# Moving the first products with v, the division and the MLP groups in an attention and mixture-of-experts kernel

## The chip, the cores and the metric

The kernel runs on one core of a Trainium2 chip. The metric is the device time of one execution in microseconds (us). A core has five engines that run their own instruction streams and meet through semaphores: TensorE (PE in the profile, its weight loads PEld) multiplies matrices, VectorE (DVE) and ScalarE (ACT) work on tiles and empty the accumulators (PSUM), GpSimd (POOL) works on tiles in SBUF, SyncE (SP) issues transfers (DMAs). Each engine works through its stream in the order in which the program writes it: an instruction that waits holds up all that stand behind it on that engine.

## The reference, cut to what matters

```python
# attention: B, H, S, D = 4, 8, 576, 64; a query sees the keys of its own and earlier blocks of 64
scores = q @ k.T / sqrt(D)          # masked with -1e9
attn   = exp(scores - max); attn /= attn.sum(-1) + 1e-9
x      = (attn @ v)                 # then laid out as 2304 tokens x 512
# first MLP, 512 -> 2048 -> 512
h = x @ w_in; x2 = maximum(0.01 * h, h) @ w_out
# mixture of experts, 8 experts, 512 -> 1024 -> 512, one expert a token, or none
out = x2;  out[t] += gate[t] * (relu(x2[t] @ w1[e]) @ w2[e])
```

## The kernel before

The change lies in the first of three stages, which takes the first 298 us: attention, with a part of the first MLP between its pieces so that TensorE has work while other engines answer. Then follow the rest of the MLP and the experts, which the change leaves as they are.

Attention runs over 16 pairs of heads. A pair has nine units of query rows: for either head the query tiles 0 to 3 (128 to 512 score columns), and between them, as unit 4, the tail of both heads (576 columns). For each unit PE makes the scores (`scores`, line 1598), DVE takes the maximum (line 1249), ACT the exponentials with their sums (`exponential`, line 1025), PE turns the result (`transposes`, line 1631), DVE or for units 3 and 8 ACT copies the turned tile out (`copy_turned`, lines 1252 and 1074). Per pair, PE multiplies with v in two halves (`p_v`, line 1643), both in one PSUM bank `ps_o`; DVE copies each half out (`copy_o`, line 1269); the sums' reciprocals are turned on PE (`turn_inverse`, line 1671, into that bank too, so it waits for the first half's copy), copied, stored by SP and spread over the partitions by SP (`spread_inverse`, line 670). POOL divides (`normalise`, line 865), ACT takes the high part (`high_x`, line 1013) and POOL the low part (`low_x`, line 872) of the quotient for the MLP. From pair 6 on, keys too are split in a high and a low part: DVE makes the high part, POOL the low part of the lower half (`low_k`, line 857), and SP copies the high part beside it (`copy_k`, line 662, DMA at 664); the scores of units 0 and 4 wait for both.

The MLP's first product is cut into groups of 12 matmuls, in two parts of 6 (`hidden`, line 1677), each product taken three times with high and low parts. Groups 0 to 31 have 512 columns, 32 to 47 have 256. A group is accumulated in a PSUM bank, ACT copies it out (`copy_hidden`, line 1042), SP stores it (`store_hidden`, line 694). Until group `TWO_BANKS` all groups share one bank, so a group's first matmul waits until ACT has copied the one before (`hidden_waits`, line 1689). Group 0 waits for pair 3's low part, and group 48, the first behind attention, for the last pair's.

The order is written out by hand as 156 steps, one for each unit and twelve more. `fill_steps` (line 118) says in which step each group's parts stand. Up to step 85 (`DOUBLE` is 86) PE does in step s the scores of unit s+2, the transposes of unit s-2, the products with v if it is their turn, and the group's part if there is one. From step 86 on two steps are taken at a time (a double step, named here by its first, as D118): PE does the scores of s+2 and s+3, the transposes of s-2 and s-1, the products with v, then the group. ACT, DVE, POOL and SP walk over the same steps; SP's loop stores in step s the groups that step s-1 completed, behind that step's other transfers.

Of the kernel before, what the change touches and what calls it, by code (L numbers as in the profile page):

```python
# [75 lines left out]
TWO_BANKS = 2 * FC + 8  # L76
# [41 lines left out]
def fill_steps():  # L118

    at = {s: [] for s in range(STEPS)}  # L120
    for g in range(N_ATT_HID):
        for part in range(2):
            if g < FC:
                s = 50 + 34 * (2 * g + part) // (2 * FC)
            elif g < 2 * FC:
                s = DOUBLE + 34 * (g - FC) // FC
            elif g < TWO_BANKS:
                s = 122 + 22 * (g - 2 * FC) // (TWO_BANKS - 2 * FC)
            else:
                s = N_UNITS + 5 + 7 * (g - TWO_BANKS) // (N_ATT_HID - TWO_BANKS)  # L130
            at[s].append((g, part))
    return at
# [13 lines left out]
def head_step(s):  # L146


    return divmod(s, UNITS) if s < DOUBLE else divmod(s - 1, UNITS) if s > DOUBLE else (N_PAIRS, 0)

# [83 lines left out]
def build(nc, q_t, k_t, v_r, w_in, w_out, w_gs, w1, w2, out):  # L234
    ctx = ExitStack()
    with ctx:
# [575 lines left out]
        def _(e):  # L812
# [74 lines left out]
            for s in range(STEPS):  # L887
# [7 lines left out]
                if i == 7 and 1 <= p <= N_PAIRS:  # L895
                    normalise(p - 1)
                if i == (3 if p < ROW_PAIRS else 1) and 2 <= p <= N_PAIRS + 1:
                    low_x(p - 2)
# [104 lines left out]
        def _(e):  # L1003
# [77 lines left out]
            def between(s):  # L1081
# [7 lines left out]
                if i == (2 if p < ROW_PAIRS else 0) and 2 <= p <= N_PAIRS + 1:  # L1089
                    high_x(p - 2)  # L1090
# [4 lines left out]
            for s in range(DOUBLE + 2):  # L1095
                if s >= 3 and s - 3 < DOUBLE - 2 and (s - 3) % UNITS in by_act((s - 3) // UNITS):
                    copy_turned(s - 3)
                if s <= DOUBLE:
                    for g in filled_at(s - 1):
                        copy_hidden(g)  # L1100
                exponential(s)
                between(s)
# [113 lines left out]
        def _(e):  # L1216
# [106 lines left out]
            for s in range(DOUBLE, STEPS, 2):  # L1323
                for u in (s + 2, s + 3):
                    if u < N_UNITS:
                        maximum(u)
                for u in (s - 2, s - 1):
                    if u < N_UNITS and u % UNITS not in by_act(u // UNITS):
                        copy_turned(u)
                for u in (s, s + 1):  # L1330
                    p, i = divmod(u, UNITS)
                    part = p_v_at(u)
                    if part and part[3] == (QT if part[1] else 2):
                        copy_o(part[0], part[1])
# [229 lines left out]
        def _(e):  # L1564
# [160 lines left out]
            for s in range(DOUBLE, STEPS, 2):  # L1725
# [4 lines left out]
                for g in before:  # L1730
                    for part in range(2):
                        hidden(g, part)
                for u in (s - 2, s - 1):
                    if u < N_UNITS:
                        transposes(u)
                products_with_v(s)
                products_with_v(s + 1)
# [258 lines left out]
```

How the kernel before makes its waits and increments, by code:

```python
        def turned(e, u):  # L541
            p, i = divmod(u, UNITS)
            act_done = 2 * p + sum(k <= i for k in by_act(p))
            dve_done = (UNITS + 1) * p + i + 1 + (i > TAIL) - act_done
            if act_done:
                e.wait_ge(s_pta, act_done)
            if dve_done:
                e.wait_ge(s_ptd, dve_done)
# [20 lines left out]
        def turned_ready(e, u):  # L570
            p = u // UNITS
            e.wait_ge(s_ptr, u + 1)
            if p >= 2:
                e.wait_ge(s_pv, 2 * (p - 1))
# [4 lines left out]
        def loaded_to(e, x, n):  # L580
            for k, loaded in enumerate(s_w[x % NW]):
                e.wait_ge(loaded, 16 * (W_LOADS // 2 * (x // NW) + (n + 2 - k) // 2))
# [1 line left out]
        def loaded_second(e, second, n):  # L585
            for k, loaded in enumerate(s_w[(E - 1) % NW]):
                e.wait_ge(loaded, second * (16 * ((n + 2 - k) // 2)) + 16 * (W_LOADS // 2))
# [19 lines left out]
        def tile_starts(e):  # L608
            e.wait_ge(s_count, 1)
            return [tile_start(e, x) for x in range(E + 1)]
# [7 lines left out]
        def load_q(e, p):  # L618
            if p >= 2:
                e.wait_ge(s_score, UNITS * (p - 1))
            e.dma_start(q_sb[p % 2][:, :], pair_in(q_t, p)).then_inc(s_qk[p % 2], 16)
# [1 line left out]
        def load_k(e, p):  # L623
            if p >= 2:
                e.wait_ge(s_score, UNITS * (p - 1))
            e.dma_start(k_sb[p % 2][:, :], pair_in(k_t, p)).then_inc(s_qk[p % 2], 16)
# [53 lines left out]
            def load_w_in(f):  # L680
                if f == 0:
                    e.wait_ge(s_maskd, 32)
                if f >= 2:
```

## Time and profile before

| | |
|---|---|
| median of 3 runs (lowest, highest) | 763.32 us (762.51, 764.35) |
| the profiled execution's own time | 763.2 us |
| its span | 761.4 us |
| granted TensorE clock | 0.999 of full speed |

The span is the time from the first to the last instruction of the program in the profile. PE's records of matmuls overlap: one with 512 columns is given some 0.39 us, while the next starts 0.23 us later. A stall is therefore better read from one start to the next than from the idle time alone, which counts from the modelled end.

### The profile page before, as it was taken

What the parts mean: (1) busy time and instruction counts of PE and PEld (TensorE: products, weight loads), DVE (VectorE), ACT (ScalarE), POOL (GpSimd) and SP (SyncE); (2) the same over time, 40 slices, a digit from 0 to 9 for tenths busy, and PEclk for the clock granted to TensorE, in tenths of its full rate; (3) what the DMA queues carried; (4) which work ended last, traced back from release to release, by engine and by line L of the source; (5) the groups of instructions that cost most, each with busy time, mean ns of one, the idle gap of its engine ahead of it and who ended that gap; (6) DMA issues with size and microseconds to landing.
All of it is one profiled execution on the core that took longest, in us unless ns stands there. A gap on an engine that the chain in (4) does not pass through costs nothing.

```text
span 761.4 us, 12875 instructions
## 1 busy us (share of the span) xinstructions
PE 741.8 (97%) x4446; PEld 597.1 (78%) x4447; DVE 359.2 (47%) x761; ACT 295.2 (39%) x685; POOL 146.5 (19%) x190
## 2 busy tenths in 40 slices
PE   7999999999999989999999999999999999999997
PEld 4555778778788778888888888888887879999984
DVE  6776454464446650122245455564556252262641
ACT  5566564465355542333322222222222131242550
POOL 3226555233212422000020000000000031212221
PEclk9999999999999999999999999999999999999999
DMA  4335677545554514556556565566653117877771
GB/s 130 115 111 158 201 217 206 155 136 141 148 150 134 158 52 122 171 147 171 159 176 189 153 179 167 186 173 172 173 160 105 56 29 238 255 237 238 229 229 58
DMA packets 97538, 121.62 MB, mean 160 GB/s; under 512 B 13842, under 2 KB 60706, under 8 KB 97480
## 3 DMA queue, kind: packets, MB, share of 16 engines
q1 hardware_dynamic: 94664, 116.50, 52.5%
q0 software_dynamic: 1920, 3.77, 1.6%
q8 instruction: 34, 0.56, 0.3%
q10 hardware_dynamic: 896, 0.59, 0.2%
q14 instruction: 24, 0.20, 0.1%
HBM read 89.09 MB, written 31.31 MB: 158 GB/s over the span
## 4 chain that ended last, share of the span: by engine, by line
PE 93%; issue 2%; ACT 1%; DVE 1%; DMA 1%; POOL 1%; SPq 0%; POOLq 0%; DVEq 0%; ACTq 0%
PE ps_h L1683 9%; PE ps_x L1760 9%; PE ps_h L1685 9%; PE ps_h L1684 9%; PE ps_x L1762 9%; PE ps_x L1761 9%; PE ps_hid L1927 8%; PE ps_o L1666 6%; PE ps_t L1640 4%; PE ps_y L1939 2%; PE ps_y L1940 2%; PE ps_y L1938 2%; PE ps_s L1627 2%; PE ps_s L1628 2%; PE ps_s L1591 1%
## 5 line engine op out<-in xcount | busy, mean ns | idle before, releaser
L1683 PE MATMUL ps_h<-xh,win_h 128*128 128x512 f32 (+1 forms) x320 | 123.4, 386 | 3.1 <-ACT act L1046 2.1
L1685 PE MATMUL ps_h<-xh,win_l 128*128 128x512 f32 (+1 forms) x320 | 118.2, 369 | 0.0
L1684 PE MATMUL ps_h<-xl,win_h 128*128 128x512 f32 (+1 forms) x320 | 118.1, 369 | 0.0
L1760 PE MATMUL ps_x<-wout_h,g_hi 128*128 128x512 f32 x288 | 114.7, 398 | 0.0
L1762 PE MATMUL ps_x<-wout_h,g_lo 128*128 128x512 f32 x288 | 112.4, 390 | 0.0
L1761 PE MATMUL ps_x<-wout_l,g_hi 128*128 128x512 f32 x288 | 112.2, 390 | 0.0
L1032 ACT ACTIVATE prob<-ps_s,neg_max 128x128 f32<-128x128 f32 (+3 forms) x144 | 78.9, 549 | 47.3 <-DVE neg_max L1249 36.2
L1046 ACT ACTIVATE act<-ps_h 128x512 f32<-128x512 f32 (+1 forms) x80 | 44.4, 554 | 135.1 <-PE ps_h L1685 135.0
L1249 DVE TENSOR_REDUCE neg_max<-ps_s 128x1 f32<-128x128 f32 (+3 forms) x144 | 71.1, 510 | 51.5 <-PE ps_s L1628 27.6
L1289 DVE TENSOR_TENSOR g_lo<-g_raw,g_hi 128x512 fp32r<-128x512 f32 x72 | 49.6, 689 | 75.8 <-ACT g_hi L1056 75.7
L1683 PEld LDWEIGHTS ps_h<-xh,win_h 128*128 128x128 f32 x320 | 60.3, 188 | 16.1 <-issue 5.9
L1685 PEld LDWEIGHTS ps_h<-xh,win_l 128*128 128x128 f32 x320 | 60.3, 188 | 10.6
L1684 PEld LDWEIGHTS ps_h<-xl,win_h 128*128 128x128 f32 x320 | 60.4, 189 | 8.5
L1760 PEld LDWEIGHTS ps_x<-wout_h,g_hi 128*128 128x128 f32 x288 | 54.1, 188 | 12.3 <-issue 2.0
L1762 PEld LDWEIGHTS ps_x<-wout_h,g_lo 128*128 128x128 f32 x288 | 54.1, 188 | 11.5
L1761 PEld LDWEIGHTS ps_x<-wout_l,g_hi 128*128 128x128 f32 x288 | 54.1, 188 | 10.4
L1056 ACT ACTIVATE g_hi<-g_raw 128x512 fp32r<-128x512 f32 x72 | 43.6, 629 | 47.4 <-PE ps_x L1762 26.9
L1255 DVE COPY pt<-ps_t 128x384 f32<-128x384 f32 (+4 forms) x113 | 46.7, 433 | 28.3 <-PE ps_t L1640 28.1
L1640 PE MATMUL ps_t<-ident,prob 128*128 128x128 f32 x339 | 54.5, 277 | 0.7 <-DVE pt L1255 0.4
L1284 DVE SCALAR_TENSOR_TENSOR g_raw<-g_raw 128x512 f32<-128x512 f32 x72 | 49.2, 684 | 7.4 <-DMA g_raw<-hidden 7.4
L1666 PE MATMUL ps_o<-pt,v_sb 128*64 128x320 f32 (+4 forms) x448 | 51.7, 365 | 0.0
L1640 PEld LDWEIGHTS ps_t<-ident,prob 128*128 128x128 f32 x339 | 39.7, 141 | 10.9 <-issue 4.1
(205 smaller groups left out, 1077.0 us busy)
## 6 DMA issues: line engine op xcount, KB each, us to landing
g_raw<-hidden SPq DMA_DIRECT2D x72, 256.0 KB, 3.8
hidden<-act SPq DMA_DIRECT2D x64, 256.0 KB, 2.4
w_sb<-in_w SPq DMA_DIRECT2D x32, 512.0 KB, 5.0
w_two<-in_w SPq DMA_DIRECT2D x32, 512.0 KB, 5.2
k_raw<-in_k_t SPq DMA_DIRECT2D x40, 144.0 KB, 3.1
x2rows<-x SPq DMA_DIRECT2D x18, 256.0 KB, 2.4
out<-x SPq DMA_DIRECT2D x18, 256.0 KB, 2.6
w_stage<-in_w_in SPq DMA_DIRECT2D x16, 256.0 KB, 3.2
```

Of the source, the lines that this page charges most:

```text
L1032: e.activation(prob_of(u), score_out(u), ACT.Exp, bias=neg_max[:, u % 4:u % 4 + 1], scale=1.0, accum_out=row_sum[p % 2][:, sum_column(u):s ...
L1249: e.tensor_reduce(out=neg_max[:, u % 4:u % 4 + 1], in_=src, axis=AX.XY if u % UNITS == TAIL else AX.X, op=ALU.max, negate=True).then_inc(s ...
L1289: e.tensor_tensor(g_lo[j % G_RING][:, :, :], g_raw[j % RAW_RING][:, :, :], g_hi[j % G_RING][:, :, :].bitcast(F32), ALU.subtract).then_inc( ...
L1640: last = e.transpose(t_bank(u, P, P * kt, P * kt + P), tile[:, P * kt:P * kt + P], ident[:, :])
L1666: last = e.matmul(ps_o[own, a:a + cols], v_sb[p % 2][:, kt, own], pt[p % 2][:, h, at:at + cols], start=kt == 0, stop=kt == tiles - 1)
L1683: e.matmul(dst, win_h[:, f, kc, :], xh[m][:, kc, :], start=kc == 0, stop=False)
L1684: e.matmul(dst, win_h[:, f, kc, :], xl[m][:, kc, :], start=False, stop=False)
L1685: last = e.matmul(dst, win_l[:, f, kc, :], xh[m][:, kc, :], start=False, stop=kc == KC - 1)
L1760: e.matmul(dst, hi, wout_h[:, f, :], start=f == 0, stop=False)
L1761: e.matmul(dst, hi, wout_l[:, f, :], start=False, stop=False)
L1762: last = e.matmul(dst, lo, wout_h[:, f, :], start=False, stop=f == FC - 1)
L1927: last = e.matmul(ps_hid[half][:, P * f - HALF * half:P * (f + 1) - HALF * half], w1_sb[i][:, c, P * f:P * f + P], rows_t[:, c, :], start= ...
```

## The change

It has five edits. (1) In double steps PE does a pair's first half of the products with v (`first_half`) in front of the transposes, and DVE copies that half out in front of the turned tiles. (2) The first 16 groups begin at step 51 instead of 50 and end at step 84 instead of 82; their parts skip steps 62 and 74 where they skipped 66. (3) `TWO_BANKS` goes from 40 to 44: groups 34 to 43 stand in one double step each (D126 to D144), where D128, D136, D142 and D144 had none, and 44 to 47 are left for the last steps instead of 40 to 47; 40 to 43 use the one bank. (4) Up to step 87 ACT takes a step's exponential in front of the copy of the group that was completed the step before. (5) In double steps POOL's division comes one step later and so behind `low_k`, and high and low part of the quotient one step later too.

```diff
--- before.py
+++ after.py
@@ -73,7 +73,7 @@
 WIDE = (0, 512, 1024, 1280, 1792, 2304)
 N_HID = (len(WIDE) - 1) * FC
 N_ATT_HID = 3 * FC
-TWO_BANKS = 2 * FC + 8
+TWO_BANKS = 2 * FC + 12
 ACT_RING = 3
 PIECE = 4
 PIECES = NT * FC // PIECE
@@ -121,11 +121,11 @@
     for g in range(N_ATT_HID):
         for part in range(2):
             if g < FC:
-                s = 50 + 34 * (2 * g + part) // (2 * FC)
+                s = 51 + 35 * (2 * g + part) // (2 * FC)
             elif g < 2 * FC:
                 s = DOUBLE + 34 * (g - FC) // FC
             elif g < TWO_BANKS:
-                s = 122 + 22 * (g - 2 * FC) // (TWO_BANKS - 2 * FC)
+                s = 122 + 2 * (g - 2 * FC)
             else:
                 s = N_UNITS + 5 + 7 * (g - TWO_BANKS) // (N_ATT_HID - TWO_BANKS)
             at[s].append((g, part))
@@ -147,6 +147,11 @@
 
 
     return divmod(s, UNITS) if s < DOUBLE else divmod(s - 1, UNITS) if s > DOUBLE else (N_PAIRS, 0)
+
+
+def first_half(s):
+
+    return p_v_at(s) is not None and p_v_at(s)[1] == 0
 
 
 def t_index(u):
@@ -892,9 +897,9 @@
                         low_k(2 * hp + 2)
                     if hi == 7:
                         low_k(2 * hp + 3)
-                if i == 7 and 1 <= p <= N_PAIRS:
+                if i == (7 if s < DOUBLE else 8) and 1 <= p <= N_PAIRS:
                     normalise(p - 1)
-                if i == (3 if p < ROW_PAIRS else 1) and 2 <= p <= N_PAIRS + 1:
+                if i == (3 if p < ROW_PAIRS else 1 if s < DOUBLE else 2) and 2 <= p <= N_PAIRS + 1:
                     low_x(p - 2)
                 f, odd = divmod(s - 42, 2)
                 if odd == 0 and 0 <= f < FC:
@@ -1086,7 +1091,7 @@
                         high_q(2 * hp + 2)
                     if hi == 7:
                         high_q(2 * hp + 3)
-                if i == (2 if p < ROW_PAIRS else 0) and 2 <= p <= N_PAIRS + 1:
+                if i == (2 if p < ROW_PAIRS else 0 if s < DOUBLE else 1) and 2 <= p <= N_PAIRS + 1:
                     high_x(p - 2)
                 f, odd = divmod(s - 42, 2)
                 if odd == 0 and 0 <= f < FC:
@@ -1095,10 +1100,10 @@
             for s in range(DOUBLE + 2):
                 if s >= 3 and s - 3 < DOUBLE - 2 and (s - 3) % UNITS in by_act((s - 3) // UNITS):
                     copy_turned(s - 3)
+                exponential(s)
                 if s <= DOUBLE:
                     for g in filled_at(s - 1):
                         copy_hidden(g)
-                exponential(s)
                 between(s)
 
 
@@ -1324,14 +1329,17 @@
                 for u in (s + 2, s + 3):
                     if u < N_UNITS:
                         maximum(u)
+                for u in (s, s + 1):
+                    if first_half(u):
+                        copy_o(p_v_at(u)[0], 0)
                 for u in (s - 2, s - 1):
                     if u < N_UNITS and u % UNITS not in by_act(u // UNITS):
                         copy_turned(u)
                 for u in (s, s + 1):
                     p, i = divmod(u, UNITS)
                     part = p_v_at(u)
-                    if part and part[3] == (QT if part[1] else 2):
-                        copy_o(part[0], part[1])
+                    if part and part[1] and part[3] == QT:
+                        copy_o(part[0], 1)
                     if i == 1 and 1 <= p <= N_PAIRS:
                         copy_inverse(p - 1)
                 between(s + 2)
@@ -1730,11 +1738,16 @@
                 for g in before:
                     for part in range(2):
                         hidden(g, part)
+
+                for u in (s, s + 1):
+                    if first_half(u):
+                        products_with_v(u)
                 for u in (s - 2, s - 1):
                     if u < N_UNITS:
                         transposes(u)
-                products_with_v(s)
-                products_with_v(s + 1)
+                for u in (s, s + 1):
+                    if not first_half(u):
+                        products_with_v(u)
                 for g in behind:
                     for part in range(2):
                         hidden(g, part)
```

Below, what the streams hold at three places. PE at steps 50 to 52: `ps_h` is a group's bank, `ps_t` holds transposes, `ps_s<-k_sb` and `ps_s<-k_st` scores. Before:

```order
L1666 MATMUL ps_o<-pt,v_sb 64x192 x2
L1666 MATMUL ps_o<-pt,v_sb 64x64 x2
L1683 MATMUL ps_h<-xh,win_h 128x512
L1684 MATMUL ps_h<-xl,win_h 128x512
L1685 MATMUL ps_h<-xh,win_l 128x512
L1683 MATMUL ps_h<-xh,win_h 128x512
L1684 MATMUL ps_h<-xl,win_h 128x512
L1685 MATMUL ps_h<-xh,win_l 128x512
L1640 MATMUL ps_t<-ident,prob 128x128 x4
L1591 MATMUL ps_s<-k_sb,q_sb 128x512 x2
L1594 MATMUL ps_s<-mask_k,mask_q 128x64 x2
```

Now:

```order
L1674 MATMUL ps_o<-pt,v_sb 64x192 x2
L1674 MATMUL ps_o<-pt,v_sb 64x64 x2
L1648 MATMUL ps_t<-ident,prob 128x128 x4
L1599 MATMUL ps_s<-k_sb,q_sb 128x512 x2
L1602 MATMUL ps_s<-mask_k,mask_q 128x64 x2
L1691 MATMUL ps_h<-xh,win_h 128x512
L1692 MATMUL ps_h<-xl,win_h 128x512
L1693 MATMUL ps_h<-xh,win_l 128x512
L1691 MATMUL ps_h<-xh,win_h 128x512
L1692 MATMUL ps_h<-xl,win_h 128x512
L1693 MATMUL ps_h<-xh,win_l 128x512
L1635 MATMUL ps_s<-k_st,q_hi 128x128
```

The first part of group 0 has moved behind step 51's scores, and the first scores with split keys (`k_st`) now follow one part and not two.

SP at steps 130 to 136: `k<-k_st` is `copy_k`, `hidden<-act` a group's store, `v_sb` the last load of v. Before:

```order
L664 DMA k<-k_st 64x576
L676 DMA inv_all<-inverse 64x576
L677 DMA inv_all<-inverse 64x64
L678 DMA inv_all<-inverse 64x512
L698 DMA hidden<-act 128x2x128
L655 DMA v_sb<-in_v_r 128x4x128
L657 DMA v_sb<-in_v_r 64x128
L664 DMA k<-k_st 64x576
L698 DMA hidden<-act 128x2x128 x2
```

Now:

```order
L669 DMA k<-k_st 64x576
L681 DMA inv_all<-inverse 64x576
L682 DMA inv_all<-inverse 64x64
L683 DMA inv_all<-inverse 64x512
L703 DMA hidden<-act 128x2x128
L660 DMA v_sb<-in_v_r 128x4x128
L662 DMA v_sb<-in_v_r 64x128
L703 DMA hidden<-act 128x2x128
L669 DMA k<-k_st 64x576
L703 DMA hidden<-act 128x2x128 x2
```

The store of group 37 now stands in front of the last `copy_k`.

ACT from D140 to the end of attention: `xh<-inv_all` is `high_x`, `act<-ps_h` the copy of a group, `pt<-ps_t` the copy of a turned tile. Before:

```order
L1046 ACTIVATE act<-ps_h 128x256
L1032 ACTIVATE prob,row_sum<-ps_s,neg_max 128x512
L1023 ACTIVATE row_sum<-row_sum 128x9
L1018 ACTIVATE xh<-inv_all 128x64
L1018 ACTIVATE xh<-inv_all 128x512
L1077 ACTIVATE pt<-ps_t 128x4x128
L1046 ACTIVATE act<-ps_h 128x256 x3
```

Now:

```order
L1051 ACTIVATE act<-ps_h 128x256
L1037 ACTIVATE prob,row_sum<-ps_s,neg_max 128x512
L1028 ACTIVATE row_sum<-row_sum 128x9
L1023 ACTIVATE xh<-inv_all 128x64
L1023 ACTIVATE xh<-inv_all 128x512
L1051 ACTIVATE act<-ps_h 128x256
L1082 ACTIVATE pt<-ps_t 128x4x128
L1051 ACTIVATE act<-ps_h 128x256 x3
```

A group's copy, that of group 42, now stands behind pair 14's high part, where no group was waiting before.

## Rows read from the trace of the kernel before

**Rows 1.** The page: busy time of each engine over the span.

```profile
PE 741.8 (97%) x4446; PEld 597.1 (78%) x4447; DVE 359.2 (47%) x761; ACT 295.2 (39%) x685; POOL 146.5 (19%) x190
```

**Rows 2.** Waits of PE, 50 to 160 us: who, for whom: us in total, times, longest.

```profile
PE ps_h L1683 <- ACT act L1046: 1.6, 5, 0.4
PE ps_s L1627 <- ACT prob L1032: 0.9, 1, 0.9
```

**Rows 3.** Waits of PE, 160 to 298 us, same columns.

```profile
PE ps_o L1675 <- DVE o_f L1274: 1.9, 3, 0.6
PE ps_s L1617 <- issue: 1.1, 2, 0.7
PE ps_h L1683 <- ACT act L1046: 0.5, 1, 0.5
PE ps_t L1640 <- DVE pt L1255: 0.4, 1, 0.4
```

**Rows 4.** PE's timeline, steps 50 to 52: start us, us, what [idle before <-releaser].

```profile
67.45 1.20 PE L1666 MATMUL ps_o<-pt,v_sb 128*64 128x320 f32 x12
69.44 0.47 PE L1683 MATMUL ps_h<-xh,win_h 128*128 128x512 f32 x1 [0.79 <-POOL xl L876]
...
70.91 0.60 PE L1640 MATMUL ps_t<-ident,prob 128*128 128x128 f32 x4
...
74.03 0.22 PE L1627 MATMUL ps_s<-k_st,q_hi 128*128 128x128 f32 x1
```

**Rows 5.** SyncE's copies of the keys, line 664: the first one, and all twenty.

```profile
L664 SPq DMA_DIRECT2D k<-k_st x1: 595/595/595, 69.6 to 69.6; - x1
DMA to landing us min/median/max: 4.0/4.0/4.0
...
DMA to landing us min/median/max: 2.3/2.9/4.0
```

**Rows 6.** PE's timeline at step 71, columns as before.

```profile
122.41 0.28 PE L1627 MATMUL ps_s<-k_st,q_hi 128*128 128x256 f32 x1
...
122.66 0.38 PE L1640 MATMUL ps_t<-ident,prob 128*128 128x128 f32 x2
123.35 0.47 PE L1683 MATMUL ps_h<-xh,win_h 128*128 128x512 f32 x1 [0.32 <-ACT act L1046]
```

**Rows 7.** PE's timeline, double steps 126 to 136.

```profile
252.14 0.39 PE L1683 MATMUL ps_h<-xh,win_h 128*128 128x256 f32 x1
...
253.67 0.27 PE L1675 MATMUL ps_o<-ident,inv 128*9 128x128 f32 x1
254.61 0.76 PE L1617 MATMUL ps_s<-k_st,q_hi 128*128 128x288 f32 x4 [0.67 <-issue]
...
257.62 0.44 PE L1627 MATMUL ps_s<-k_st,q_hi 128*128 128x384 f32 x1 [0.95 <-ACT prob L1032]
...
269.23 0.70 PE L1617 MATMUL ps_s<-k_st,q_hi 128*128 128x288 f32 x4
```

**Rows 8.** SyncE's issue of the last copy of line 664 (timeline).

```profile
265.60 0.48 SPq L664 DMA_DIRECT2D k<-k_st  x1
```

**Rows 9.** ScalarE's timeline, double step 132.

```profile
266.14 0.76 ACT L1018 ACTIVATE xh<-inv_all 128x64 fp32r<-128x64 f32 x2
266.81 0.36 ACT L1046 ACTIVATE act<-ps_h 128x256 f32<-128x256 f32 x1
```

**Rows 10.** ScalarE's timeline, double step 142.

```profile
284.24 0.78 ACT L1018 ACTIVATE xh<-inv_all 128x64 fp32r<-128x64 f32 x2 [2.24 <-POOL inv_all L869]
```

**Rows 11.** GpSimd's timeline, the last pair's low part.

```profile
292.76 1.75 POOL L876 TENSOR_TENSOR xl<-inv_all,xh 128x64 fp32r<-128x64 f32 x2 [0.43 <-ACT xh L1018]
```

**Rows 12.** PE's timeline, D140's start, the last turn_inverse, the first group behind attention.

```profile
277.37 0.34 PE L1627 MATMUL ps_s<-k_st,q_hi 128*128 128x384 f32 x1
...
283.93 0.27 PE L1675 MATMUL ps_o<-ident,inv 128*9 128x128 f32 x1 [0.62 <-DVE o_f L1274]
...
297.94 0.40 PE L1683 MATMUL ps_h<-xh,win_h 128*128 128x512 f32 x1
```

## The prediction, made before the changed kernel was run

> **What bounds the kernel now.** I read the page first: PE is busy for 97% of the span [rows 1], so the end is set by PE and time can only come from its stalls. The change touches nothing behind 298 us, and adds or removes no work at all: it moves instructions. So I read PE's waits in the two stretches that it reorders. From 50 to 160 us (steps up to 85) the largest is for ACT's copies of MLP groups, five waits with 1.6 us in all, then one for an exponential [rows 2]. From 160 to 298 us (double steps) it is three waits for the first half's copy out of `ps_o`, then `issue`, a group's copy and a turned tile [rows 3]. Then I followed PE's timeline start to start at each of them, because the idle time of a row is too small: at step 71 two transposes of some 0.11 each start at 122.66, the next matmul at 123.35, so 0.47 us are lost where the row says 0.32 [rows 6]. All the waits of [rows 2, 3] and the one in [rows 4], with 0.16 to 0.25 us added to each, are 9 to 10 us: that is what a perfect order could win.
>
> **Steps 50 to 85.** Group 0 now begins one step later. Step 50's products with v start at 67.45 and take 1.20, and the group's first matmul waits until 69.44 [rows 4]: 1.0 us lost (0.79 as idle time), and covered in future by step 51's transposes and scores, which need only results that are there. What is late next are the first scores with split keys, at 74.03 [rows 4]. They wait for SP's copy of the key, which was issued at 69.6 and landed 4.0 us later, at 73.6 [rows 5]: before they had 0.4 us of slack. SP issues its transfers back to back there and does not follow PE. Now PE gets there at 68.6, plus the 3.1 us from 70.91 to 74.03 (transposes, scores and one part) is 71.7, and waits 1.9 us. Net of the two: +0.9. The landing is the unknown: at the 2.3 us of the fastest copy [rows 5] the wait is 0.2 and the net -0.8. I take 4.0, since it is this very transfer with the same traffic around it.
>
> The page "DMA: Bandwidth & Descriptors" of the Trainium skill, section "Anatomy of one DMA", gives a transfer about 2.0 us of fixed cost and bytes over 436 GB/s on top; for 64 x 576 words that would be an estimate of 2.3 us. The fastest of the twenty agrees, this one took 4.0 [rows 5]; by the page the change would gain here and not lose, which is the second rival below.
>
> The waits for a group's copy. From a part's last product to the next group's first matmul at least 0.94 us pass (122.41 to 123.35 in [rows 6]: the last product drains, ACT copies, PE goes on). What stands between them hides it or not: some 1.1 us and more at the positions 1, 2 and 4 in a pair (much scoring, or products with v), 0.3 to 0.8 us at the others. Groups began at even steps up to 64 and at odd ones from 67; eight of these boundaries are short, and lose 1.6 + 5 x 0.16 and three under the profile's threshold with 0.6 us in all: 3.0. Now they begin at 53, 55, 57, 59, 61, 64, 66, 68, 70, 72, 75, 77, 79, 81 and 83; short are 53 (0.45 missing), 61 (0.6), 66 (0.55), 68 (0.25), 70 (0.6), 72 (0.35), 77 (0.15), 79 (0.55) and 81 (0.3): 3.8. So +0.8. The copy itself is not later, though the exponential now stands in front of it: ACT idles for the group's end there, and does the exponential in that time.
>
> That earlier exponential ends the 0.9 us wait (1.1 start to start) of `scores` behind the empty step 66 [rows 2], which has a part now; steps 62 and 74 become empty in its place, and their exponentials are done a step sooner. I take -1.1 and for step 84, whose emptiness costs 0.2, -0.2; if the new empty steps cost as much as the old, it is +1.1. Sum of this stretch: +0.9 + 0.8 - 1.3 = +0.4, between -1.4 and +2.8.
>
> **Double steps up to D134.** A half in front of the transposes lets DVE's copy run beside these. In D118, which has no group, it takes 0.6 us off the first of the three `ps_o` waits. It is worth nothing: at 254.61, in D128, PE waits for another copy of a key (`issue`, 0.67) [rows 7], whose place in SP's back-to-back queue does not move, and arrives 0.6 us earlier to wait 0.6 us longer. Elsewhere the half stands in a step with a group, and nothing waited. The price is that exponentials which wait for a transpose come 0.9 us later; they have a double step of slack. The group that is new in D128 takes 1.5 us (252.14 to 253.67 [rows 7]) and covers the wait that ends at 257.62 (0.95 idle, 1.2 start to start [rows 7]): -1.2. In D134 PE waited 0.5 us for a group's copy (0.65 start to start) [rows 3] because ACT took pair 13's high part first, 0.76 us [rows 9]; this moves behind the next exponentials: -0.6.
>
> The division behind `low_k` costs nothing by itself: its quotient is needed four or more steps later, and `low_k`, 3 us earlier now, wasn't late either.
>
> **D136.** Here SP's order bites. The last `copy_k` was issued at 265.60 [rows 8], and the scores that need it started at 269.23 [rows 7], 0.2 us behind its landing. Now the store of group 37 is in front of it in SP's queue, and waits for ACT's copy. That copy starts at 266.81 before [rows 9], and at 266.3 without the high part in front; it takes 0.36, the store 0.4: `copy_k` is issued at 267.2 and, at the median landing of 2.9 [rows 5], there at 270.1. PE, by then 0.4 us ahead, wants it at 268.8: +1.3, between +0.6 (2.3 us) and +2.4 (4.0 us). Behind the SP queue stands nothing that is urgent.
>
> The wait for `o_f` in D136, 0.85 start to start, goes behind transposes and group: -0.8.
>
> **D142 and D144.** A turned tile (0.45 idle, 0.6) and the third `o_f` wait (0.85) [rows 3] go: -1.4. But in D142 ACT waited 2.24 us for pair 14's division before its high part [rows 10], and group 42's copy now stands behind that; group 43 must wait for it in their one bank. The high part ends at 284.24 + 0.78 = 285.0 [rows 10], 7.7 us behind D140's first scores at 277.37 [rows 12]; the copy behind it (0.36) is done 8.0 us behind them, and PE goes on 0.1 later. PE wants it when D140 and D142 are through: 6.6 us from 277.37 to 283.93 less the 1.4 that go, plus group 42's 1.5 and 0.2 of the turn, 6.9. So +1.2 (0 to +1.6).
>
> **The end of attention.** Up to the last pair's `turn_inverse` the stalls sum to -1.2 - 0.6 + 1.3 - 0.8 - 1.4 + 1.2 = -1.5. But four groups more stand in front of it, 4 x 1.5: it moves from 283.93 [rows 12] to 288.4. From there a chain of its own runs: copy, store, spread, division, high part, low part. It ended 10.6 us behind 283.93, at 294.5 (292.76 + 1.75) [rows 11], while PE worked off groups 40 to 47 and started group 48 at 297.94 [rows 12]: 3.4 us of slack. Now the chain ends at 288.4 + 10.6 = 299.0. PE has only 0.7 for the inverse's copy, 2.2 of products with v and four groups, 6.1, and is done at 297.4: a new wait of 1.6 us for `xl`. Group 48 starts at 299.1, or +1.1. So the double steps gain 1.5 and the end takes this back: without the four groups as cover the chain sets the end.
>
> **Sum.** 0.4 + 1.1 = +1.5 us on the profiled execution's 763.2 (span 761.4 and 1.8 around it). The median is 0.1 higher, and the small joints that I rounded off (empty steps cost some 0.1 each at their ends) add 0.1 or 0.2: 763.3 + 1.7 = 765.0 us. What this kernel's measurement can tell from no change is 0.2%, 1.5 us: the forecast lies just beyond.
>
> **Rivals.** (a) The stalls only trade places and the two landings come a little earlier: 763.3, no change. For it: all terms are of one size and both signs. Against it: both key copies had under 0.5 us of slack and lose more than that. (b) Not slower but faster: the copies of keys land in 2.3 us. Place: step 52 and D136. Then step 52 costs 1.7 less and D136 0.7 less, and 765.0 - 2.4 = 762.6; if also group 37's store is not late, since SP is ahead, D136 costs nothing and it is 762.0. It decides at a landing of some 3 us. For it: the median is 2.9. Against: the first took 4.0. By the Trainium skill's estimate of 2.3 us for a copy, the forecast would be this rival. (c) Clearly slower: the new empty steps 62 and 74 wait for exponentials as 66 did, +2.2, 767.2. For it: same place in the order; against it: ACT has the exponential first now. (d) The new order doesn't change the stalls of D118 to D144, because ACT and not PE's order sets them: the four groups then cost their full length until the chain, +1.5 more, 766.5. Against it: these waits are latencies of one copy, and ACT is half idle.
>
> **Chances.** Forecast 0.38, (a) 0.22, (b) 0.22, (c) 0.08, (d) 0.10. Three quarters of the forecast's own spread, (c) and (d) are beyond +0.2%, as said: slower 0.46. Most of (b) reaches -1.3 us at most, which is within 0.2%; a part of it with smaller waits for copies is beyond: faster 0.17, within 0.2% 0.37. The range takes in (b)'s lower part and (c): 761.2 to 767.4; the forecast's own is 764.0 to 766.2.
>
> **What would show it.** Right: a wait of PE's first split scores of 1 to 2 us near 71.7; the idle time before L1675 gone; a wait of scores for `issue` above 1 us in D136; a new wait of PE for `xl` of 1 to 2 us in front of group 48; a wait for `act` in D144. Wrong: group 48's start below 298, or landings of 2.3 at step 52.

## The result

The changed kernel takes 764.74 us (median of 13 runs, 764.02 to 766.92), the kernel before 763.32 (13 runs beside them). The ratio is 1.0025, with a 95% interval of 1.0017 to 1.0034: 1.9 us slower, 1.3 to 2.6. The forecast was 765.0 and slower by more than 0.2%.

The profiled execution of the changed kernel took 766.92 us (span 765.2), the slowest of the 13, against 763.2 (span 761.4). So the traces differ by 3.7 us where the medians differ by 1.4, and I first split off what isn't the change. The first `turn_inverse` of a pair starts at 16.55 us, against 16.00 before, though nothing up to there is changed. In the twelve experiments below this start lies between 15.57 and 16.38. That 0.55 is the execution's own. A second part, 1.6 us, is a fall of the clock at 300 us, shown below. What is left is 3.7 - 0.55 - 1.6, some 1.6 us.

The page, first row of the engines:

```profile
PE 744.1 (97%) x4446; PEld 598.4 (78%) x4447; DVE 359.9 (47%) x761; ACT 295.6 (39%) x685; POOL 145.9 (19%) x190
```

The counts are those of [rows 1], so no work was added. PE's waits from 50 to 160 us, the answer to [rows 2]:

```profile
PE ps_h L1691 <- ACT act L1051: 2.2, 6, 0.5
PE ps_s L1635 <- issue: 1.2, 1, 1.2
```

And from 160 to 302 us, the answer to [rows 3]:

```profile
PE ps_h L1691 <- POOL xl L881: 1.8, 1, 1.8
PE ps_s L1625 <- issue: 1.5, 1, 1.5
PE ps_s L1625 <- DVE q L1245: 0.8, 1, 0.8
PE ps_h L1691 <- ACT act L1051: 0.8, 1, 0.8
PE ps_o L1674 <- DVE inv_t L1272: 0.5, 1, 0.5
PE ps_s L1635 <- ACT prob L1037: 0.5, 1, 0.5
```

The two waits for an exponential of 0.9 us and those for the first half's copy `o_f` are gone, and so are the one for group 0's low part [rows 4] and the one for the turned tile. Six that were not there have come: for the key's copy at step 52, for an exponential in D120 (0.5), for `q`, for group 42's copy, for `inv_t`, and for the last pair's low part. The wait for a key's copy in D98 (the 1.5 for `issue`) was there and has grown. PE's timeline at step 52, the answer to [rows 4], columns as there:

```profile
72.28 0.40 PE L1693 MATMUL ps_h<-xh,win_l 128*128 128x512 f32 x1
73.86 0.30 PE L1635 MATMUL ps_s<-k_st,q_hi 128*128 128x128 f32 x1 [1.18 <-issue]
```

PE's timeline from D144 to the first group behind attention, the answer to [rows 12]:

```profile
287.71 0.38 PE L1691 MATMUL ps_h<-xh,win_h 128*128 128x256 f32 x1 [0.84 <-ACT act L1051]
...
289.24 0.27 PE L1683 MATMUL ps_o<-ident,inv 128*9 128x128 f32 x1
289.97 2.27 PE L1674 MATMUL ps_o<-pt,v_sb 128*64 128x320 f32 x20 [0.46 <-DVE inv_t L1272]
...
299.95 0.50 PE L1691 MATMUL ps_h<-xh,win_h 128*128 128x512 f32 x1 [1.76 <-POOL xl L881]
```

ScalarE's timeline shows group 42's copy behind pair 14's high part, the answer to [rows 10]:

```profile
286.61 0.77 ACT L1023 ACTIVATE xh<-inv_all 128x64 fp32r<-128x64 f32 x2 [2.29 <-POOL inv_all L874]
287.29 0.36 ACT L1051 ACTIVATE act<-ps_h 128x256 f32<-128x256 f32 x1
```

The last pair's turn comes 5.3 us later than before, and group 48 2.0 us later. From the turn to group 48 it is 10.7 us, where it was 14.0 before. GpSimd's timeline shows who holds it, the answer to [rows 11]:

```profile
296.32 1.43 POOL L874 TENSOR_TENSOR inv_all<-o_f,inv_all 128x576 f32<-128x576 f32 x1 [7.57 <-DMA inv_all<-inverse]
298.18 1.72 POOL L881 TENSOR_TENSOR xl<-inv_all,xh 128x64 fp32r<-128x64 f32 x2 [0.43 <-ACT xh L1023]
```

The low part ends at 299.90, and PE starts at once. Behind that wait PE's granted clock was at half. The table by stretch (us, then busy time and instructions of PE, PEld, DVE, ACT and POOL, then granted clock, DMA share and GB/s):

```profile
294.00:298.00 4.00, 4.00 (x35) 3.98 (x34) 0.00 (x0) 0.90 (x4) 1.43 (x1) 1.00 0.38 104
298.00:302.00 4.00, 2.24 (x8) 1.62 (x7) 0.00 (x0) 1.10 (x4) 1.58 (x2) 0.79 0.43 108
302.00:306.00 4.00, 4.00 (x16) 3.22 (x15) 0.00 (x0) 1.12 (x2) 0.00 (x0) 0.78 0.74 226
```

In PE's timeline there, start to start of matmuls of 512 columns is 0.43 us:

```profile
300.64 0.63 PE L1693 MATMUL ps_h<-xh,win_l 128*128 128x512 f32 x1
301.07 0.63 PE L1691 MATMUL ps_h<-xh,win_h 128*128 128x512 f32 x1
...
304.16 0.39 PE L1693 MATMUL ps_h<-xh,win_l 128*128 128x512 f32 x1
304.39 0.39 PE L1691 MATMUL ps_h<-xh,win_h 128*128 128x512 f32 x1
```

At 304 it is 0.23 again. In windows of 0.5 us the granted clock is 0.50 (1.2 instead of 2.4 GHz) from 300.45 to 303.45. The matmuls between 300.29 and 303.9 took 1.6 us more than at the full rate.

### The profile page after: what moved, and what is told of

Same layout as the page of the kernel before. It is cut to its first block, busy times and chain, and to the rows that moved or that the text cites. A ratio compares the mean times of both kernels' runs of the same rounds, so it can differ in the third digit from the quotient of the medians.

```text
span 765.2 us, 12875 instructions
## 1 busy us (share of the span) xinstructions
PE 744.1 (97%) x4446; PEld 598.4 (78%) x4447; DVE 359.9 (47%) x761; ACT 295.6 (39%) x685; POOL 145.9 (19%) x190
## 4 chain that ended last, share of the span: by engine, by line
PE 89%; DMA 3%; issue 2%; SPq 2%; ACT 1%; DVE 1%; POOL 1%; POOLq 0%; DVEq 0%; ACTq 0%
PE ps_x L1773 9%; PE ps_h L1691 9%; PE ps_x L1775 9%; PE ps_x L1774 9%; PE ps_hid L1940 8%; PE ps_h L1693 8%; PE ps_h L1692 8%; PE ps_o L1674 5%; PE ps_t L1648 4%; PE ps_y L1952 2%; PE ps_y L1953 2%; PE ps_y L1951 2%; PE ps_s L1636 1%; PE ps_s L1635 1%; PE ps_s L1599 1%
## 5 line engine op out<-in xcount | busy, mean ns | idle before, releaser
L1693 PEld LDWEIGHTS ps_h<-xh,win_l 128*128 128x128 f32 x320 | 60.6, 189 | 10.6
L1774 PEld LDWEIGHTS ps_x<-wout_l,g_hi 128*128 128x128 f32 x288 | 54.1, 188 | 10.4
```

The costliest lines, as they stand in the source:

```text
L1693: last = e.matmul(dst, win_l[:, f, kc, :], xh[m][:, kc, :], start=False, stop=kc == KC - 1)
L1774: e.matmul(dst, hi, wout_l[:, f, :], start=False, stop=False)
```

## The experiments

The experiments fall into three groups, each on one chip beside its own executions of the kernel before, and ratios are against those. A difference between two experiments of different groups is a difference of such ratios. "Before" and "changed" are the two kernels of this case.

**Half of the edits each.** First the edits of the single steps alone (2 and 4), then those of the double steps alone (1, 3, 5).

```diff
 # b_single, against before
-                s = 50 + 34 * (2 * g + part) // (2 * FC)
+                s = 51 + 35 * (2 * g + part) // (2 * FC)
+                exponential(s)
                 if s <= DOUBLE:
                     for g in filled_at(s - 1):
                         copy_hidden(g)
-                exponential(s)
```

> Before with edits 2 and 4 alone (groups 0 to 15 from step 51, exponential in front of the group's copy up to step 87); the double steps stay as before. My theory (most of the loss stands at the end of attention): no wait in front of group 48, and within 0.6 us of before, with the wait for the copy of a key at step 52 (1.35 us in the changed kernel) and the empty step's exponential gone. Rival (the stretch up to step 85 carries the loss): 1.5 us or more slower than before.

Measured: 763.75 us, ratio 1.0012 (1.0001 to 1.0023), so +0.9 us. No wait in front of group 48; the wait at step 52 is 1.56 us. The 0.9 is more than my 0.6, and by the interval it is 0.1 to 1.8 us. In its trace, with 0.35 us taken off for its later start (16.35), the turn at 172.83 comes 0.3 us later than before and the one at 198.20 0.9 us later: the larger part of the loss lies not in the steps that the edits reorder but in D98, where the wait for a key's copy grew.

> Before with edits 1, 3 and 5 alone; up to step 85 as before. My theory: 1.2 to 2.0 us slower than before, PE waits 1.8 +- 0.4 us for xl in front of group 48, though the last turn of the inverse comes some 1 us earlier than groups moved ahead of it explain. Rival (that wait is only the profile's, the double steps gain): 1 us faster than before, no wait for xl.

Measured: 763.78, ratio 1.0008 (1.0000 to 1.0017), +0.6 us, less than I expected. PE's waits of this kernel, 160 to 302 us:

```profile
PE ps_h L1691 <- POOL xl L881: 1.5, 1, 1.5
PE ps_s L1625 <- DVE q L1245: 0.8, 1, 0.8
PE ps_h L1691 <- ACT act L1051: 0.6, 1, 0.6
PE ps_s L1625 <- issue: 0.5, 1, 0.5
```

The wait for `xl` is there, 1.5 us, and it comes from the double steps alone. The last turn starts at 287.62 (3.69 us later than before, for 5.76 us of moved groups; its start was 0.24 us earlier), so the double steps did gain, some 1.8 us, and the end took it back. The two halves, +0.9 and +0.6, are 1.5 of the 1.9 us.

**How many groups stand in front of the last turn.** `TWO_BANKS` at 42 and at 40, where the changed kernel has 44.

```diff
 # a_tb42 (a_tb40), against the changed kernel
-TWO_BANKS = 2 * FC + 12
+TWO_BANKS = 2 * FC + 10      # a_tb40: + 8
```

> The changed kernel with TWO_BANKS 42: groups 42 and 43 move from D142 and D144 behind attention again, all else stays. They give PE 3 us more of work beside the chain of 10.6 us. My theory: the wait of 1.8 us for xl in front of group 48 is gone, that for group 42's copy (1.0) too, so 2 to 3 us faster than the changed kernel and 0.5 to 1.5 faster than before. Rival (the chain does not set the end): same time as the changed kernel.

> The changed kernel with TWO_BANKS 40: groups 40 to 43 behind attention as before, 34 to 39 at D126 to D136. My theory: no wait for xl, 3 us of slack unused; D138 to D144 without groups give 0.5 to 1 us of stalls back, so within 0.7 us of the kernel with 42. Rival (every group moved ahead costs its length): 3 us faster than with 42.

Measured: 42 gives 763.31, ratio 1.0007 (0.9995 to 1.0018), 40 gives 762.01, ratio 0.9988 (0.9980 to 0.9997). The wait for `xl` is gone in both, as the chain demands. But 42 did not beat before: a wait that I had not expected took its place. PE's and ScalarE's timelines of that kernel:

```profile
287.36 2.27 PE L1674 MATMUL ps_o<-pt,v_sb 128*64 128x320 f32 x20 [1.65 <-ACT pt L1082]
```

```profile
286.05 0.78 ACT L1023 ACTIVATE xh<-inv_all 128x64 fp32r<-128x64 f32 x2 [2.06 <-POOL inv_all L874]
286.73 0.58 ACT L1082 ACTIVATE pt<-ps_t 128x512 f32<-128x512 f32 x1
```

ScalarE stands for 2.06 us in front of pair 14's high part, and the last turned tile is queued behind it. At 44, two groups more kept PE busy in that time. At 40 D148 holds two groups and not one, and half of a double step's groups stand in front of its products with v (`groups_at`, line 140): PE has group 40 to do between the turn (282.69) and those products, and only idle times of 0.92 (an exponential) and 0.73 us (`issue`, in front of products with v) are left from D138 on. With one group in D148, as at 42 and 44, nothing stands between: that is also why the changed kernel waits for `inv_t`, the 0.7 us that the prediction has for the inverse's copy. So pair 14 has such a chain too, and it holds whatever is queued behind its members. a_tb40 is faster than both kernels of this case, by 0.9 us against before (0.2 to 1.5) on its chip.

**The high part behind the turned tile.**

```diff
 # a_tb42_hx, against a_tb42 (ScalarE's loop)
-                if i == (2 if p < ROW_PAIRS else 0 if s < DOUBLE else 1) and 2 <= p <= N_PAIRS + 1:
+                if i == (2 if p < ROW_PAIRS else 0 if s < DOUBLE else 2 if p == N_PAIRS else 1) and 2 <= p <= N_PAIRS + 1:
                     high_x(p - 2)
```

> The changed kernel with TWO_BANKS 42 and ScalarE's high part of pair 14's quotient one double step later, behind the last turned tile. With 42 alone PE waits 1.9 us in front of the last products with v for a turned tile that ScalarE copies behind this high part, which itself waits 2.1 us for the division. My theory (the pair's own chain of 10.6 us holds ScalarE's queue): that wait is gone, 1.2 to 1.9 us faster than with 42 alone, which had +0.5 against before. Rival (the turned tile is late by itself): no change.

Measured: 762.03, ratio 0.9991 (0.9980 to 1.0001), 1.2 us better than 42 alone by the ratios, at the lower end of what I expected. The wait is 0.58 us: ScalarE's copy of the tile starts as soon as PE has turned it (287.49) and ends at 288.09.

```profile
288.14 2.16 PE L1674 MATMUL ps_o<-pt,v_sb 128*64 128x320 f32 x16 [0.58 <-ACT pt L1082]
```

**Who holds D136.** In the changed kernel two things that PE needs are ready within 0.1 us of each other, VectorE's low part of the queries and SyncE's copy of the key. VectorE's, GpSimd's, SyncE's and PE's timelines:

```profile
268.57 1.85 DVE L1245 SCALAR_TENSOR_TENSOR q<-q_raw,q_hi 64x640 fp32r<-64x640 f32 x1
```

```profile
266.81 1.42 POOL L866 TENSOR_TENSOR k_st<-k_raw,k_st 64x576 fp32r<-64x576 f32 x1 [6.61 <-DVE k_st L1240]
268.31 1.43 POOL L874 TENSOR_TENSOR inv_all<-o_f,inv_all 128x576 f32<-128x576 f32 x1
```

```profile
268.04 0.48 SPq L669 DMA_DIRECT2D k<-k_st  x1
```

```profile
270.68 0.51 PE L1625 MATMUL ps_s<-k_st,q_hi 128*128 128x288 f32 x2 [0.84 <-DVE q L1245]
```

The copy of the key is issued right behind the store of group 37 and landed 2.33 us later, at 270.36. VectorE's low part of the queries ended at 270.42. PE was ready for both at 269.66, when the matmul of 512 columns that starts at 269.43 had had its 0.23. Undone one by one and together:

```diff
 # a_div, against the changed kernel (GpSimd's loop; high and low part one step sooner too)
-                if i == (7 if s < DOUBLE else 8) and 1 <= p <= N_PAIRS:
+                if i == 7 and 1 <= p <= N_PAIRS:
                     normalise(p - 1)
 # a_copyk, against the changed kernel (SyncE's loop); a_div_copyk has both
-                    if hi == 7 and ROW_PAIRS <= hp + 1 < N_PAIRS:
+                    if hi == (6 if hp == N_PAIRS - 2 else 7) and ROW_PAIRS <= hp + 1 < N_PAIRS:
                         copy_k(2 * hp + 3)
```

> The changed kernel with edit 5 undone (division in front of low_k, high and low part of the quotient one step sooner in double steps). In the changed kernel PE waits 1.0 us in front of D136's scores; the last copy of a key landed at 270.36, and VectorE's low part of the queries ended at 270.42, 1.85 us long where it takes 0.81 elsewhere, because it started inside GpSimd's division. My theory (two causes end together): VectorE's instruction takes 0.81 us again, but PE still waits, now for the copy's landing: 0.8 to 1.1 us. Rival (the division alone makes the wait): it is gone.

> The changed kernel with the last copy_k one step sooner in SP's queue, in front of the store of group 37. My theory: it is issued some 1.3 us sooner, at the end of VectorE's cast, but PE waits as before, 0.8 to 1.1 us, for VectorE's low part of the queries (1.85 us long). Rival (the store alone makes the wait, as the prediction had it): it is gone.

> Both edits: division in front of low_k, last copy_k in front of the store. My theory: the wait at D136 is gone (under 0.3 us), and with the same 1.0 us less in front of it the end of attention comes 1 us sooner: total 0.7 to 1.3 us faster than the changed kernel. Rival (a third thing holds D136's scores): a wait of 0.8 us stays.

Measured, the rows of PE in D134 and D136. a_div:

```profile
267.45 0.39 PE L1691 MATMUL ps_h<-xh,win_h 128*128 128x256 f32 x1 [1.27 <-ACT act L1051]
270.24 0.77 PE L1625 MATMUL ps_s<-k_st,q_hi 128*128 128x288 f32 x4 [0.62 <-issue]
```

a_copyk:

```profile
271.33 0.77 PE L1625 MATMUL ps_s<-k_st,q_hi 128*128 128x288 f32 x4 [0.84 <-DVE q L1245]
```

a_div_copyk, which has no idle time above 0.3 us in front of D136's scores:

```profile
270.33 0.38 PE L1691 MATMUL ps_h<-xh,win_h 128*128 128x256 f32 x1 [1.26 <-ACT act L1051]
```

a_copyk is a clean test of one side: the store is out of the copy's way, and the wait of 0.84 us stays, so `q` alone holds PE as long. The other side rests on the changed kernel's own trace, where the key landed 0.06 us before `q` was done. a_div and a_div_copyk don't isolate it. With edit 5 undone the high part of pair 13 stands in front of group 37's copy again, and PE waits 1.27 us for that copy in D134, the place where [rows 3] had 0.5. So PE comes 1.3 us later to D136, which hides most of what it could wait for there. In a_div the store, and behind it the key's copy, is also issued later (267.83, 2.7 us behind the start of D134's scores with 384 columns at 265.12, where it was 1.3 in the changed kernel).

I was wrong on `q`: in a_div it took not 0.81 but 1.54 us, now inside `low_k`, so by these two traces edit 5's own share of the lengthening from 0.81 to 1.85 is 0.3 us. GpSimd's timeline of a_div:

```profile
264.53 1.79 POOL L874 TENSOR_TENSOR inv_all<-o_f,inv_all 128x576 f32<-128x576 f32 x1 [5.94 <-DMA inv_all<-inverse]
266.40 1.41 POOL L866 TENSOR_TENSOR k_st<-k_raw,k_st 64x576 fp32r<-64x576 f32 x1
```

The division starts 0.6 us before D134's scores with 384 columns, where it was 2.4 us before them in the kernel before (263.21 to 265.66), because the spread lands later. SyncE issues the store of the turned sums 4.5 us behind VectorE's copy of them (254.12 to 258.59; 255.65 to 260.13 in the changed kernel), where it was 3.2 before (253.97 to 257.21): in the changed kernel SyncE stands for 2.5 us (253.79 to 256.32) at two groups' stores ahead of it. That this is the price of the stores that edit 3 brought there is read from the rows, not tested.

Undoing edit 5 costs at the end too: in a_div group 48 started 11.9 us behind the last turn, since PE waited 2.12 us for a group's copy queued behind the last high part, and the clock fell behind that wait. The times: a_div 767.07 and a_copyk 765.78 (one execution each, which settles nothing about their times), a_div_copyk 767.15, ratio 1.0051 (1.0034 to 1.0069), slower than the changed kernel where I expected 0.7 to 1.3 us faster. Its profiled execution also had a wait of 2.32 us at D98 with a fall of the clock behind it, which no edit of it touches. Its six executions stand apart by the clock: two at a mean clock of 0.999 took 764.43 and 764.54, near the changed kernel, and four at 0.995 or 0.996 took 766.87 to 768.57. So how much of its loss is edit 5's order and how much such falls is not shown.

**Copies of keys one step sooner.**

```diff
 # a_sooner, against the changed kernel (SyncE's loop, the same for hi == 7)
+COPY_SOONER = (12, 13, 16, 17, 21, 22, 23, 25, 29, 30, 31)
-                    if hi == 3 and ROW_PAIRS <= hp + 1 < N_PAIRS:
+                    if hi == 3 - (2 * hp + 2 in COPY_SOONER) and ROW_PAIRS <= hp + 1 < N_PAIRS:
                         copy_k(2 * hp + 2)
```

> The changed kernel with eleven copies of keys one step sooner in SP's queue (the 12th, 13th, 16th, 17th, 21st to 23rd, 25th and 29th to 31st split head, whose casts were done 1.4 to 5.9 us before SP issued them). In the changed kernel PE waits 1.4 us at step 52 and 1.7 at D98 for such a landing. My theory (SP's queue, not the cast, makes these landings late): both waits fall by 1 us or more; 2 to 3 us faster than the changed kernel. Rival (the landing takes as long as the traffic lets it, whenever issued): the same waits, no gain.

Measured: 763.94, ratio 1.0012 (1.0003 to 1.0021), by the ratios 1.0 us better than the changed kernel, where I expected 2 to 3. At step 52 the wait stayed (1.26 us): the copy was issued at 70.24, hardly sooner, since it is still behind a load of queries. At D98 it fell from 1.54 to 0.67. Here the rows of issue (of the changed kernel, then of a_sooner) and of PE's scores (in the same order):

```profile
190.35 0.51 SPq L669 DMA_DIRECT2D k<-k_st  x1
```

```profile
188.65 0.59 SPq L670 DMA_DIRECT2D k<-k_st  x1
```

```profile
194.21 0.63 PE L1625 MATMUL ps_s<-k_st,q_hi 128*128 128x288 f32 x3 [1.54 <-issue]
```

```profile
192.72 0.77 PE L1626 MATMUL ps_s<-k_st,q_hi 128*128 128x288 f32 x4 [0.67 <-issue]
```

Issued 1.0 us before the kernel before issued it (189.64), this copy landed at 192.63, where that one landed at 192.67. In a_busy and best_tb40 it was issued at 188.85 and 188.92, and landed at 192.65 and 192.64. In these, issuing it sooner brought nothing, as the rival has it. But it is no rule: in a_div_copyk it was issued at 189.09 and landed 5.0 us later, in b_double at 189.75 and 3.0 us later. That traffic sets the landing is an argument; what sets it is not shown.

**All together**, to beat both kernels, with 42 and with 40.

```diff
 # best1 (best_tb40: TWO_BANKS + 8), against the changed kernel
-TWO_BANKS = 2 * FC + 12
+TWO_BANKS = 2 * FC + 10
 # ScalarE's line of a_tb42_hx and SyncE's two lines of a_sooner, and in GpSimd's loop
-                if i == (7 if s < DOUBLE else 8) and 1 <= p <= N_PAIRS:
+                if i == 7 and 1 <= p <= N_PAIRS:
                     normalise(p - 1)
```

Of edit 5 only the division's place is undone here; the low part stays one step later, the high part too, that of pair 14 two.

> The changed kernel with TWO_BANKS 42, the eleven copies sooner, ScalarE's high part of pair 14 one double step later, and GpSimd's division in front of low_k again. My theory: gains of the single edits add up (0.5 against before for 42, -1.3 to -1.9, -2 to -3, -0.5): 3 to 4 us faster than before, 759 to 760 us. Rival (they hide each other behind the last pair's chain): a new wait for xl of 1 us or more, and under 2 us faster than before.

> As best1, with TWO_BANKS 40. My theory: two groups more stand beside the last pair's chain, so no wait for xl, but D142 and D144 keep their stalls of 0.9 to 1.1 us: within 1 us of best1. Rival: 1.5 us or more faster than best1, if the chain still limits that one.

Measured: best1 762.98, ratio 1.0007 (0.9994 to 1.0020); best_tb40 763.40, ratio 1.0008 (0.9998 to 1.0018). Neither is shown to be faster than before, where I expected 3 to 4 us of best1, and by the ratios neither beats a_tb40. The largest wait from 160 to 302 us of best1 (best_tb40 has 1.7 at the same place):

```profile
PE ps_s L1626 <- POOL k_st L867: 1.5, 1, 1.5
```

That is D136 again: the low part of the key is late, and a wait of 0.8 us has become 1.5 to 1.7. GpSimd's timeline of best1:

```profile
266.73 1.43 POOL L875 TENSOR_TENSOR inv_all<-o_f,inv_all 128x576 f32<-128x576 f32 x1 [7.72 <-DMA inv_all<-inverse]
268.24 1.86 POOL L867 TENSOR_TENSOR k_st<-k_raw,k_st 64x576 fp32r<-64x576 f32 x1
```

It takes both edits. In a_div the division is in front as well, but starts at 264.53, and the low part ends at 267.81 and nobody waits for it. Here SyncE issues the copy of a key before the store of the turned sums (259.02 and 259.66; 259.55 and 258.59 in a_div), the spread follows 1.3 us later (262.81, 261.49), and the division that waits for it holds `low_k` until 270.10. So copies of keys one step sooner and the division in front of `low_k` don't go together. With `low_k` first, `low_k` does not wait for the spread; a version of this kind with edit 5 kept was not run.

**Work in the place of the last wait.**

```diff
 # a_busy, against the changed kernel
+            for i in range(8):
+                e.matmul(ps_t[:, 0:BANK], win_h[:, 0, 0, :], xh[0][:, 0, :], start=True, stop=True)
             for g in range(N_ATT_HID, N_HID):
```

> The changed kernel with eight more matmuls (128x512, results unused) in front of group 48, 1.8 us of work in the time in which PE waits for xl. In the profiled execution of the changed kernel PE's clock stood at half for some 3 us behind this wait of 1.8 us. My theory (PE's idle time makes the clock fall): group 48 starts at the same time, the clock stays at full, and the median is 0 to 1 us lower than the changed kernel's, without its executions above 766. Rival (the clock falls for another reason): the fall stays, same time or slower.

Measured: PE's timeline and the table by stretch.

```profile
296.35 2.00 PE L1759 MATMUL ps_t<-xh,win_h 128*128 128x512 f32 x8
298.28 0.50 PE L1691 MATMUL ps_h<-xh,win_h 128*128 128x512 f32 x1
```

```profile
298.00:302.00 4.00, 4.00 (x18) 3.09 (x17) 0.00 (x0) 0.49 (x2) 0.22 (x1) 1.00 0.50 117
```

Group 48 starts 10.7 us behind the last turn (287.56), as in the changed kernel: the chain, not PE, sets it. The clock stays at full, and the profiled execution took 763.68. But the median is 764.97 over five executions, ratio 1.0039 (1.0026 to 1.0052), with two above 766 (766.16 and 767.63, at mean clocks of 0.996 and 0.994): against what I expected the median did not fall and the long executions stayed. One trace agrees with the idea that PE's idle time makes the clock fall at this place; since waits of like length in other traces had no fall behind them (below), it does not prove it, and that the work pays is not shown.

## Why the prediction was right

What follows goes by the prediction's own steps, with measured times from the two traces and stalls start to start. Three readings of the prediction were off. Its total of stalls, 9 to 10 us, comes to 9.4 to 10.7 by its own terms, and left out the 0.95 us for an exponential in [rows 7]. Each wait for `o_f` is 0.69 and not 0.85: 1.49 from the second half's first matmul to the turn, less the 0.80 that its eight matmuls take elsewhere (151.84 to 152.64). And group 48 at 299.1 left out its own +0.4 of the steps up to 85; with that it is 299.5.

- **Group 0 covered.** 1.0 us gone, as forecast.
- **Step 52, the key's copy.** Forecast 1.9, measured 1.35 (72.28 to 73.86, less 0.23). The landing took 3.4 us and not the 4.0 that I took from the same transfer before; in the other kernels with edit 2 the wait was 0.66 to 2.3. The mechanism was right, the one number from one transfer too exact. The estimate of 2.3 us from the page "DMA: Bandwidth & Descriptors" of the Trainium skill did not come true here; its section "Anatomy of one DMA" gives these figures for transfers that GpSimd issues, and this one is SyncE's. The last copy, at 268.04, did take 2.33.
- **Groups' copies.** Forecast +0.8, from nine short boundaries. Measured 2.7 and 3.8 over the waits above 0.24, +1.1. Seven of the nine boundaries show; 68 and 77 don't, and step 55, 0.70 us, was not on my list.
- **Exponentials.** 1.1 and 0.2 us gone, and the new empty steps 62 and 74 wait for nothing: rival (c) fell. I can't say which of edits 2 and 4 did it; they were not run apart.
- **D98: missed.** The wait for the key's copy grew from 0.56 to 1.70. I had taken landings outside step 52 and D136 as unchanged. b_double, with the first 85 steps as before, has 0.65; the nine kernels with edit 2 or 4 and this copy at its old place have 1.1 to 2.5. So edits 2 and 4 move it, not those of the double steps; through which transfers, stays open.
- **D118 to D130.** Forecast: 0.6 off at D118 and given back at 254.61. In fact 0.55 is off at D118 (first scores to turn: 3.65 before, 3.10 now) and 0.62 lost to a new wait for an exponential in D120, where I had counted on slack; and both waits behind it, 0.9 in D128 and 1.1 in D130, are gone, where I had expected only the second to go.
- **D134.** -0.6 forecast, -0.67 measured.
- **D136.** Forecast +1.3 for the key's copy behind the store, measured 1.0. The copy was ready 0.06 us before `q`, and a_copyk shows that moving it away would not have helped: `q` inside the division holds as long. This second holder is not in the prediction at all. VectorE's instruction is 1.04 us longer at the one place where nobody has slack; 0.3 of that is edit 5's, so "costs nothing by itself" is not quite true, and the rest comes with the later spread. The wait for `o_f` behind it is gone, 0.7 and not 0.8.
- **D142 and D144.** -1.3 (0.6 for the tile, 0.7 for `o_f`) where I had -1.4; +1.2 for group 42's copy behind pair 14's high part came as 1.0. Behind the last turn, `inv_t` took the 0.7 that I had for the inverse's copy.
- **Up to the last turn.** Forecast -1.1 beside the moved groups (+0.4 and -1.5). Measured: 5.31 less 5.76 (48 matmuls of 0.12) less 0.55 of the start = -1.0. But its parts differ. By the turns at 172.83, 198.20 and 283.93 of the kernel before (173.14, 199.61 and 289.24 now), the steps up to 85 gave -0.2 where I had +0.4, D98 +1.1 where I had nothing, and the double steps behind it -1.9 where I had -1.5.
- **The end.** Chain 10.6 forecast, 10.7 measured (10.4 to 10.8 in five kernels whose last wait is for `xl`, or which had work in its place). Wait 1.6 forecast, 1.76 measured. Group 48 at 299.5 forecast, with the 0.4; measured 299.95, or 299.40 without the start.

Of the signs that I had named, the wait of the first split scores, the idle time gone before the turn, the wait for `xl` and the one for `act` in D144 came. The wait of D136's scores for `issue` above 1 us did not: it was 0.84, for `q`.

So the forecast of 765.0 against 764.74 was right for its main reason, the chain at the end, which b_double, a_tb42 and a_tb40 bear out. That it was right to 0.3 us is luck: D98 (+1.1) came unforecast, and steps 50 to 85 (0.6) and the double steps (0.4) were better than I took them. That the loss could be turned into a gain shows in a_tb40: the same edits, with the four groups left behind the last turn, are 0.9 us faster than before (0.2 to 1.5). The 3.4 us of slack in [rows 11, 12] were worth two groups, and the change spent four.

## What to carry to other kernels

Work that fills stalls is also cover for latency chains elsewhere: before moving it, measure the chain at its old place (here 10.6 us from turn to low part) and what remains beside it. And read every in-order queue behind the moved instruction: ScalarE's high part, SyncE's store and GpSimd's division each held something urgent that was ready and merely queued.

## What the runs showed of the hardware

**VectorE waits for GpSimd's instruction to end.** The low part of the queries, two operands in SBUF, takes 0.81 us, and 1.85 in the row above. It began at 268.57 inside GpSimd's division, which ended at 269.74, and was done 0.68 us later. In the same trace it began inside a GpSimd instruction at 68.79, 101.62, 123.89 and 165.88 as well, and ended 0.67 or 0.68 us behind it each time. The other way round, at 250.59 it began 0.03 us in front of a division, took its 0.81, and the division took 2.06 us where it takes 1.43. The Trainium skill says so ("SBUF — State Buffer", section "Who interferes with whom"): a VectorE instruction with two SBUF inputs and a GpSimd instruction that reads SBUF exclude each other, and the later one is blocked for the whole of the other. The trace agrees. I had not looked for it.

**A wait of some 2 us can cost twice.** PE's matmuls ran at 1.2 GHz for some 3.3 us, half of it lost, behind idle times of 1.62, 1.76, 1.79, 1.83, 2.12 and 2.32 us in six profiled executions. They did not behind 1.58, 1.64, 1.65, 1.68, 1.73, 1.78 and 2.09, nor behind any single one of 1.56 or less. But in best_tb40 they ran so from 282.5 to 285.6, behind two idle times of 0.92 and 0.73 us within 1.5 us; a_tb40 has the same two and no such fall. So the length of one wait does not decide it, and what does is not shown. The row of best1 and its stretch:

```profile
73.83 0.30 PE L1636 MATMUL ps_s<-k_st,q_hi 128*128 128x128 f32 x1 [1.79 <-POOL k_st L867]
```

```profile
76.00:80.00 4.00, 3.79 (x18) 2.78 (x15) 1.41 (x4) 1.79 (x7) 1.66 (x2) 0.78 0.80 235
```

This is also a likely cause for the spread of single kernels (best1: 761.36 to 766.49 us, mean clock 0.999 and 0.994 at these two, and a_div_copyk above); it is argued from the clocks of the executions, not shown one by one, and the changed kernel has one of 766.07 at a mean clock of 1.0, where it can't be the cause.
